# Sparse attention in blocks of 32 queries by 64 keys: tiles, steps and engine order of the attention stage

## The chip, the cores and the metric

The kernel runs on one core of one Trainium2 chip. The metric is the device time of one execution in microseconds. Times of the trace count from its first instruction.

## The reference

The program computes three layers one after another: a masked attention, a mixture of experts with a skip decision, and a feed-forward layer. The change touches the attention alone:

```python
# batch 4, heads 8, sequence S = 576, head_dim 64, stride 32
scores = (q @ k.T) / sqrt(64)
rel = pos[:, None] - pos[None, :]
mask_local   = (rel >= 0) & (rel < 32)                   # heads 0 to 3
mask_strided = (rel >= 0) & (pos_k % 32 == pos_q % 32)   # heads 4 to 7
scores = where(mask, scores, -1e9); scores -= max(scores)
attn = exp(scores); attn /= sum(attn) + 1e-9
out = attn @ v
```

A query of a local head sees the 32 keys up to its own. A query of a strided head sees the keys of its residue class, 18 positions of 576. After the attention, x is its output of shape 2304x512; each token goes to one of eight experts (512 to 1024 to 512) and then through a layer 512 to 2048 to 512.

## The kernel before

q and k come transposed (partition = head half and head dimension), in two orders: by position for the local heads (q_loc, k_loc), and by residue class for the strided ones (q_str, k_str), so that a class is 18 neighbours. A batch is cut into 12 tiles: six local ones of 96 queries by 128 keys and six strided ones of six or five classes (108x108 or 90x90). Two neighbouring tiles form a twin, and a step does one twin for the four heads of its kind. With four batches there are 24 steps (`STEPS`, `TB` = 6).

The work of a step goes through four engines:

1. TensorE, `scores`: four bf16 matmuls with the identity write the masks into PSUM (L806), and eight fp32 matmuls add the scores (L814). The two head halves hh lie on partitions 0 to 63 and 64 to 127, and so on two row tiles of the array.
2. VectorE, `maxima`: one reduction over PSUM for eight maxima (L604) and their scaling (L606).
3. ScalarE, `exps`: eight activations (L489), one for each tile and head, with the maximum as bias, each followed by a read of the accumulator that gives the sum.
4. VectorE, `inverses` (L611, L613); GpSimd multiplies the weights by the inverse sums, once for each tile (L407).
5. TensorE, `turn`: eight transposes (L827); VectorE copies them to SBUF (`copy_turned`, L620); TensorE, `values`: eight fp32 matmuls with v (L841); ScalarE, `place`, copies the result into XT (L497).

An fp32 matmul appears in the trace as two instructions with a weight load each, a transpose as one.

The order on each engine is written by hand: step s does the scores of s and the turning and values of s - 3 (`LAG` = 3). The first five steps and the last are unrolled; the rest is a hardware loop over batches on each engine. TensorE's order in a round is `turn(s-3)`, `scores(s)`, `values(s-3)`; ScalarE's is `exps(s)`, `place(s-3)`; VectorE's is `copy_turned(s-3)`, `maxima(s)`, `inverses(s-1)`. PSUM has two buffers for the scores, two for the turned weights and two for the values. The inputs have one buffer for each kind; SP loads the next batch's local part when the local steps are scored, and so on, by semaphores. The first q_loc and k_loc come in two pieces, so that the first step needs 192 columns of each only.

When all 24 steps are done, the logits (L868) and the rows of x (L862, L513) follow, then routing, the scatter by GpSimd, the experts and the last layer.

Of the kernel before, what the change touches and what calls it, by code (L numbers as in the profile page):

```python
# [7 lines left out]
F32 = mybir.dt.float32  # L8
# [20 lines left out]
LQ = 96  # L29
LT = S // LQ  # L30
CLASSES = [6, 6, 5, 5, 5, 5]
TILES = [(LQ, P, LQ * t, max(0, LQ * t - STRIDE), False, t) for t in range(LT)]
for _t, _c in enumerate(CLASSES):
    _o = PHASE * sum(CLASSES[:_t])
    TILES.append((PHASE * _c, PHASE * _c, _o, _o, True, _t))
TWINS = [(TILES[i], TILES[i + 1]) for i in range(0, len(TILES), 2)]
TB = len(TWINS)
LB = TB // 2
QMAX = PHASE * max(CLASSES)
# [3 lines left out]
LAG = 3  # L43
# [15 lines left out]
C_ID, C_ML0, C_ML, C_MS, C_UP, C_W8, C_TOK, C_ONE, C_END = 0, 128, 256, 384, 492, 620, 628, 646, 774  # L59
# [7 lines left out]
def program(nc, qT, kT, vl, vs, wg, w1, w2, win, wout, cst, out):  # L67
    with ExitStack() as ctx:
# [22 lines left out]
        k_loc, _, o = at("k_loc", [P, 2, S], F32, o)  # L91
        q_str, _, o = at("q_str", [P, 2, S], F32, o)
        k_str, _, o = at("k_str", [P, 2, S], F32, o)
        v_loc, _, o = at("v_loc", [P, LT, 4 * HD], F32, o)
        v_str, _, o = at("v_str", [QMAX, LT, 4 * HD], F32, o)
# [8 lines left out]
        prob, p_at, o = at("prob", [QMAX, 3, 8 * P], F32, o)  # L104
        probT, _, o = at("probT", [P, 2, 4 * QMAX], F32, o)
# [28 lines left out]
        mask_b, _, _ = at("mask_b", [P, C_UP - C_ML0], BF16)  # L134
        wgs, _, _ = at("wgs", [P, DC, LGW], F32)
        sm, _, _ = at("sm", [P, 3, 32], F32)
# [36 lines left out]
        score_b = [ctx.enter_context(nc.psum_tensor(f"pair{i}", [P, 2, 512], F32)) for i in range(2)]  # L173
        bank = [score_b[0][:, 0, :], score_b[0][:, 1, :]]
        bank += [ctx.enter_context(nc.psum_tensor(f"bank{i}", [P, 512], F32)) for i in range(2, 6)]
        bank += [score_b[1][:, 0, :], score_b[1][:, 1, :]]
        warm_b = bank[0]
        probT_b, out_b = bank[2:4], bank[4:6]
# [14 lines left out]
        qk_loc_in, v_loc_in = sem("qk_loc_in"), sem("v_loc_in")  # L193
        qk_str_in, v_str_in = sem("qk_str_in"), sem("v_str_in")
        zeroed, gate_padded, warm_ready, cast = sem("zeroed"), sem("gate_padded"), sem("warm_ready"), sem("cast")
        qk_first_in, masks_in = sem("qk_first_in"), sem("masks_in")
        scored, maxed, biased, probs_done = sem("scored"), sem("maxed"), sem("biased"), sem("probs_done")
        summed, inverted, normed, turned, turn_copied = sem("summed"), sem("inverted"), sem("normed"), sem("turned"), sem("turn_copied")
# [26 lines left out]

        STEPS = B * TB
        FIRST = LAG + 2
        LOOPS = (STEPS - FIRST) // TB

        def steps(eng, step, lag):  # L230
            for s in range(FIRST):
                step(s, s, 0)
            with eng.Fori(0, LOOPS) as b:
                for i in range(TB):
                    step(FIRST + i, TB * b + (FIRST + i), b)
            for s in range(FIRST + LOOPS * TB, STEPS + lag):
                step(s, s, 0)

# [9 lines left out]
        def x_place(i, b):  # L248

            q, _, q0, _, strided, t = TWINS[i][0]  # L250
            src = out_b[i % 2][:, 0:4 * q].rearrange("d (p r) -> d p r", p=2)
            if strided:
                c0, c = sum(CLASSES[:t]), 2 * CLASSES[t]
                dst = XT[:, 2:4, bass.ds(b * S, S)].rearrange("d p (m r) -> d p r m", r=STRIDE)[:, :, c0:c0 + c, :]
                return dst, src.rearrange("d p (r m) -> d p r m", r=c)
            return XT[:, 0:2, bass.ds(b * S + q0, 2 * q)], src

        @block.sync
        def _(sp):
# [3 lines left out]
            def load_local(b, q0=0, q1=S, k0=0, k1=S, arrived=qk_loc_in):  # L263
                sp.dma_start(q_loc[:, :, q0:q1], qT[b, 0, :, :, q0:q1]).then_inc(arrived, 16)
                sp.dma_start(k_loc[:, :, k0:k1], kT[b, 0, :, :, k0:k1]).then_inc(arrived, 16)

            def load_strided(b):
                sp.dma_start(q_str[:, :, :], qT[b, 1]).then_inc(qk_str_in, 16)
                sp.dma_start(k_str[:, :, :], kT[b, 1]).then_inc(qk_str_in, 16)

            def load_v_local(b):
                sp.dma_start(v_loc[:, :, :], vl[b]).then_inc(v_loc_in, 16)

            def load_v_strided(b):
                t0 = 0
                for c, n in ((6, 2), (5, 4)):
                    r0, r = PHASE * sum(CLASSES[:t0]), PHASE * c
                    sp.dma_start(v_str[0:r, t0:t0 + n, :], vs[b, r0:r0 + r * n].rearrange("(t p) d -> p t d", t=n)).then_inc(v_str_in, 16)
                    t0 += n

            load_local(0, q1=2 * LQ, k1=2 * LQ, arrived=qk_first_in)
            load_local(0, q0=2 * LQ, k0=2 * LQ)
            load_v_local(0)
            sp.dma_start(con[:, C_UP:C_END], cst[:, C_UP:C_END]).then_inc(con_in, 16)
            sp.dma_start(pairs[:, :], cst[0:EXTRA, C_END:C_COLS]).then_inc(pairs_in, 16)
            load_strided(0)
            load_v_strided(0)
            sp.wait_ge(zeroed, ZEROED)
# [767 lines left out]
```

## Time and profile before

| | us |
|---|---|
| median of 3 runs | 704.28 (704.14 to 705.2) |
| the profiled execution | 704.93 |
| its span, first to last instruction | 703.2 |
| PE busy | 657.1 (93%) |
| VectorE busy | 330.2 (47%) |
| ScalarE busy | 229.0 (33%) |
| GpSimd busy | 149.3 (21%) |

Busy shares are averages over the whole program. The attention stage is its first 93 us, and there the shares are others. PE stands for TensorE's matmuls, PEld for its weight loads, DVE for VectorE, ACT for ScalarE, POOL for GpSimd, SPq for the DMA queue of SyncE. PE's busy time contains the modelled end of each matmul, so its groups overlap a little. The granted clock is given as a share of 2.4 GHz.

### The profile page before, as it was taken

Reading aid. Unit: us, or ns where it says so; the run is one execution under the profiler, and the core shown is the slowest. Engines: PE = TensorE matmul, PEld = TensorE weight load, DVE = VectorE, ACT = ScalarE, POOL = GpSimd, SP = SyncE. Lnnn points to the kernel's source line nnn. Section 1 sums busy time; section 2 is a strip of 40 time slices with the busy share of each in tenths; the row PEclk is TensorE's granted clock in tenths of the full one; section 3 lists DMA queues with packets and bytes.
Section 4 is the critical chain, followed back from the end, with each engine's and each line's share of the span. In section 5 each row is a group of like instructions: output and inputs, shape, how many; then the busy total and the mean of one; then the engine's idle time right before and its main releaser. Section 6 shows DMA issues by size and latency. Waiting matters only on the chain.

```text
span 703.2 us, 11023 instructions
## 1 busy us (share of the span) xinstructions
PE 657.1 (93%) x4149; PEld 567.4 (81%) x4149; DVE 330.2 (47%) x614; ACT 229.0 (33%) x693; POOL 149.3 (21%) x163
## 2 busy tenths in 40 slices
PE   7999892299999999989999999999999999999995
PEld 4877762299999999968888888888888888888994
DVE  3877733032111112387445644456445564455653
ACT  4999932032111111122223322233222332222331
POOL 1655506302221222785000200002000020000201
PEclk8999977599999999999999999999999999999998
DMA  8565166693777776222000100001000010000100
GB/s 259 180 214 207 40 255 261 225 394 126 265 263 248 262 264 225 88 94 60 1 1 0 61 1 0 1 0 60 0 0 0 0 60 0 0 0 1 61 1 30
DMA packets 37854, 73.95 MB, mean 105 GB/s; under 512 B 2739, under 2 KB 16224, under 8 KB 37808
## 3 DMA queue, kind: packets, MB, share of 16 engines
q1 hardware_dynamic: 34936, 63.92, 26.3%
q0 software_dynamic: 2880, 9.52, 3.5%
q8 instruction: 24, 0.39, 0.2%
q14 instruction: 14, 0.11, 0.1%
HBM read 63.49 MB, written 9.94 MB: 104 GB/s over the span
## 4 chain that ended last, share of the span: by engine, by line
PE 82%; ACT 6%; DMA 4%; POOL 3%; issue 2%; DVE 2%; SPq 0%; DVEq 0%
PE pair L970 28%; PE pair L983 15%; PE bank L983 12%; PE pair L927 10%; PE bank L937 9%; ACT prob L489 5%; DMA WE<-w 2%; POOL x_sorted L418 2%; PE bank L841 1%; PE bank L827 1%; PE bank L911 1%; PE pair L814 1%; PE bank L868 1%; DMA k_loc<-kT 1%; ACT XT L497 1%
## 5 line engine op out<-in xcount | busy, mean ns | idle before, releaser
L970 PE MATMUL pair<-yh,WIH 128*128 128x512 f32 (+1 forms) x320 | 116.5, 371 | 0.2 <-ACT yh L548 0.2
L970 PE MATMUL pair<-yh,WIL 128*128 128x512 f32 (+1 forms) x320 | 116.3, 370 | 0.0
L572 ACT ACTIVATE cl<-cl,half 128x512 f32<-128x512 f32 (+1 forms) x80 | 54.5, 681 | 187.2 <-DVE cl L768 187.2
L477 POOL DMA_INDIRECT out<-XT,tok x18 | 18.8, 1045 | 351.6 <-DVE XT L756 347.7
L776 DVE TENSOR_TENSOR gl<-gr,gh 128x512 fp32r<-128x512 f32 (+1 forms) x80 | 56.3, 703 | 73.1 <-ACT gh L581 71.9
L768 DVE TENSOR_SCALAR cl<-pair 128x512 f32<-128x512 f32 (+1 forms) x80 | 50.9, 637 | 71.0 <-PE pair L970 70.8
L970 PE MATMUL pair<-yl,WIH 128*128 128x512 f32 (+1 forms) x320 | 79.9, 370 | 2.1 <-DVE yl L747 2.1
L927 PE MATMUL pair<-xw,WE 128*128 128x168 f32 x512 | 75.7, 310 | 0.3 <-DMA WE<-w 0.3
L927 PEld LDWEIGHTS pair<-xw,WE 128*128 128x128 f32 x512 | 74.5, 193 | 0.7 <-DMA WE<-w 0.6
L581 ACT CAST gh<-gr 128x512 fp32r<-128x512 f32 (+1 forms) x80 | 46.3, 578 | 85.7 <-PE bank L983 58.3
L937 PE MATMUL bank<-hid,WE 128*128 128x168 f32 x512 | 74.1, 306 | 0.0
L937 PEld LDWEIGHTS bank<-hid,WE 128*128 128x128 f32 x512 | 73.3, 190 | 0.0
L970 PEld LDWEIGHTS pair<-yh,WIH 128*128 128x128 f32 x320 | 60.8, 190 | 11.3 <-ACT yh L548 0.6
L970 PEld LDWEIGHTS pair<-yh,WIL 128*128 128x128 f32 x320 | 60.7, 190 | 10.6
L489 ACT ACTIVATE prob<-pair,sm 96x128 f32<-96x128 f32 (+2 forms) x192 | 65.7, 419 | 10.5 <-DVE sm L606 9.4
L970 PEld LDWEIGHTS pair<-yl,WIH 128*128 128x128 f32 x320 | 57.0, 189 | 13.0 <-DVE yl L747 3.1
L774 DVE TENSOR_TENSOR gr<-gr,cl 128x512 f32<-128x512 f32 (+1 forms) x80 | 52.6, 657 | 22.6 <-ACT cl L572 22.6
L983 PE MATMUL pair<-WOH,gh 128*128 128x512 f32 x160 | 62.5, 391 | 0.0
L983 PE MATMUL pair<-WOL,gh 128*128 128x512 f32 x160 | 62.4, 390 | 0.0
L983 PE MATMUL pair<-WOH,gl 128*128 128x512 f32 x160 | 62.3, 389 | 0.0
L728 DVE TENSOR_TENSOR ytmp<-bank,gb 128x168 f32<-128x168 f32 x32 | 10.6, 333 | 105.6 <-PE bank L937 105.6
L529 ACT ACTIVATE hid<-pair 128x168 f32<-128x168 f32 x64 | 19.9, 310 | 109.7 <-PE pair L927 109.7
(124 smaller groups left out, 933.7 us busy)
## 6 DMA issues: line engine op xcount, KB each, us to landing
WE<-w SPq DMA_DIRECT2D x16, 2048.0 KB, 9.1
xrow<-x_sorted SPq DMA_DIRECT2D x6, 781.5 KB, 10.5
raw_in<-win SPq DMA_DIRECT2D x16, 256.0 KB, 9.2
raw_out<-wout SPq DMA_DIRECT2D x16, 256.0 KB, 2.5
v_loc<-vl SPq DMA_DIRECT2D x4, 768.0 KB, 5.1
q_str<-qT SPq DMA_DIRECT2D x4, 576.0 KB, 5.8
k_str<-kT SPq DMA_DIRECT2D x4, 576.0 KB, 6.8
q_loc<-qT SPq DMA_DIRECT2D x3, 576.0 KB, 4.6
```

Source lines behind the costliest of these rows:

```text
L477: pool.indirect_dma_start(out, bass.IndirectOffsetOnAxis(tok[:, GT * g + t:GT * g + t + 1], 0), rows_of(g, t), None).then_inc(out_done if ...
L489: last = act.activation(prob[0:q, i % 3, e * kk:(e + 1) * kk], score_b[i % 2][0:q, e // 4, e % 4 * kk:(e % 4 + 1) * kk], ACT.Exp, bias=sm[ ...
L529: act.activation(hid[:, par, f, :], hid_b[f % 2][:, 0:WIN], ACT.Relu).then_inc(h_done, 1)
L572: act.activation(cl[:, 0:n], cl[:, 0:n], ACT.Square, bias=half[:, :], scale=0.5).then_inc(squared, 1)
L581: act.copy(gh[:, f % 2, 0:n], gr[:, 0:n]).then_inc(g_high, 1)
L768: dve.tensor_scalar(cl[:, 0:n], h2_b[f % 2][:, 0:n], -1.0, 1.0, ALU.max, ALU.min).then_inc(clamped, 1)
L774: dve.tensor_tensor(gr[:, 0:n], gr[:, 0:n], cl[:, 0:n], ALU.add).then_inc(g_ready, 1)
L776: dve.tensor_tensor(gl[:, f % 2, 0:n], gr[:, 0:n], gh[:, f % 2, 0:n].bitcast(F32), ALU.subtract).then_inc(g_low, 1)
L927: last = pe.matmul(hid_b[f % 2][:, 0:WIN], WE1[:, par, c, P * f:P * (f + 1)], xw[:, buf, c, :], start=(c == 0), stop=(c == DC - 1))
L937: last = pe.matmul(y_b[c][:, 0:WIN], WE2[:, par, f, P * c:P * (c + 1)], hid[:, par, f, :], start=(f == 0), stop=(f == FEC - 1))
L970: last = pe.matmul(h2_b[f % 2][:, 0:tokens], w[:, c, P * f:P * (f + 1)], x[:, c, 0:tokens], start=(k == 0), stop=(k == 3 * DC - 1))
L983: last = pe.matmul(fin_b[t][:, :], x[:, f % 2, P * t:P * (t + 1)], w[:, f, :], start=(f == 0 and k == 0), stop=(f == FFC - 1 and k == 2))
```

## The change

The attention stage is written anew; what follows it stays.

- Tiles. The local heads work in blocks of 32 queries with 64 keys, the strided heads in strips of three classes (54 queries) with 64 keys. Scores stand in groups of 128 rows by 64 keys: four blocks, or two strips, lie below one another. A step does two such groups (j = 0, 1) for four heads, 128 rows by 512 columns. There are five steps for each batch, 20 in all: two of strips, one with the rest (a pair of strips, the first and the last block, the first and the last class), two of blocks.
- TensorE. A step has 4 mask matmuls of 128 columns, and fp32 matmuls of 64 moved columns for the scores: 16 for strips, 24 for the rest, 32 for blocks. The blocks' outputs lie on four column tiles of 32 rows, the strips' on two of 64, and the head halves on two row tiles. The four transposes are 128x128. The values have 16, 24 or 32 matmuls on 64 partitions, with 54, 18 or 32 moved columns and 64 weight columns; the two key halves j alternate. In the rest step, the scores of the two halves are done one after the other.
- Softmax. VectorE takes the maxima and subtracts them from PSUM into prob; ScalarE does one activation of 128x512; VectorE sums, guards and inverts; GpSimd multiplies once.
- The copy of the turned weights moves from VectorE to ScalarE. Scores have three buffers, the turned weights one, prob and the small values five.
- Loads. All inputs come whole, strided first. v_str has 128 rows, v_loc 8 blocks of 128 rows, v_rest three. The batches' loads are unrolled on SP and ordered by scored and pv_done. Constants and padding writes move into the loads of batches 1 and 2.
- VectorE, ScalarE and GpSimd are unrolled; TensorE's loop goes round three times over five steps.

```diff
+TILES_OF = [
+    [(MASK_S[j], [strip(x, j, x) for x in range(2)]) for j in range(2)],
+    [(MASK_S[j], [strip(2 + x, j, x) for x in range(2)]) for j in range(2)],
+    [(MASK_X[j], rest_of_batch(j)) for j in range(2)],
+    [(MASK_L, [block(t + 2 * j, j, n) for n, t in enumerate(FIRST_BLOCKS[0:4])]) for j in range(2)],
+    [(MASK_L, [block(t + 2 * j, j, n) for n, t in enumerate(FIRST_BLOCKS[4:8])]) for j in range(2)],
+]
+SCORES_IN = [0, 1, 2, 0, 1]
...
 # SP
+            load_qk_strided(0)
+            load_qk_local(0)
+            load_v_strided(0)
+            load_v_rest(0)
             load_v_local(0)
+            for b in range(1, B):
+                done = TB * (b - 1)
+                sp.wait_ge(scored, done + REST_STEP + 1)
+                load_qk_strided(b)
+                if b > 1:
+                    sp.wait_ge(pv_done, done)
+                    load_v_local(b - 1)
+                sp.wait_ge(scored, done + TB)
+                load_qk_local(b)
+                sp.wait_ge(pv_done, done + STRIPS_B + 1)
                 load_v_strided(b)
+                sp.wait_ge(pv_done, done + REST_STEP + 1)
+                load_v_rest(b)
...
 # ScalarE
-                for e in range(8):
-                    last = act.activation(prob[0:q, i % 3, e * kk:(e + 1) * kk], score_b[i % 2][0:q, e // 4, e % 4 * kk:(e % 4 + 1) * kk], ACT.Exp,
-                                          bias=sm[0:q, i % 3, 8 + e:9 + e], scale=SCALE, accum_out=sm[0:q, i % 3, 16 + e:17 + e])
+                act.activation(prob[:, n % SLOTS, :], prob[:, n % SLOTS, :], ACT.Exp, scale=SCALE).then_inc(probs_done, 1)
+            def copy_turned(n):
+                act.wait_ge(turned, n + 1)
+                behind(act, pv_done, n)
+                act.copy(probT[:, :], probT_b[:, :]).then_inc(turn_copied, 1)
+            for s in range(STEPS + LAG):
+                if 0 <= s - 1 < STEPS:
+                    exps(s - 1)
+                if 0 <= s - LAG < STEPS:
+                    copy_turned(s - LAG)
+                    place(s - LAG)
 # VectorE
+                dve.tensor_reduce(small[:, 0:8].rearrange("q (h g) -> q h g", h=2), scores, AX_X, ALU.max).then_inc(maxed, 1)
+                dve.tensor_tensor(prob[:, n % SLOTS, :].rearrange("q (h g k) -> q h g k", g=4, h=2), scores,
+                                  small[:, 0:8]...to_broadcast([P, 2, 4, KEYS]), ALU.subtract).then_inc(lowered, 1)
+                dve.tensor_reduce(small[:, 8:16], prob[:, n % SLOTS, :].rearrange("q (g k) -> q g k", g=8), AX_X, ALU.add).then_inc(summed, 1)
+                dve.tensor_scalar(small[:, 16:24], small[:, 8:16], 1e-9, None, ALU.add).then_inc(guarded, 1)
+                dve.reciprocal(small[:, 24:32], small[:, 16:24]).then_inc(inverted, 1)
 # TensorE
+            def scores_of(i, hh):
+                for j, (mask, _) in enumerate(TILES_OF[i]):
+                    pe.matmul(out.rearrange("q (p j k) -> q p j k", p=2, j=2)[:, :, j], ident_b[:, :], mask_b[:, mask, :].unsqueeze(1).to_broadcast([P, 2, KEYS]), ...)
+                    yield
+                for j, (_, parts) in enumerate(TILES_OF[i]):
+                    for p in range(2):
+                        for x in parts:
+                            yield pe.matmul(out[x.row:x.row + x.queries, col:col + KEYS], queries[half_, p, x.first:x.first + x.queries], keys[half_, p, x.keys:x.keys + KEYS], ...)
+            def values(n, i, b):
+                for p in range(2):
                     for hh in range(2):
+                        for pair in zip(*(parts for _, parts in TILES_OF[i])):
+                            for j, x in enumerate(pair):
+                                last = pe.matmul(out_b[KEYS * hh:KEYS * (hh + 1), j, to:to + x.queries], vv[half_, x.index, HD * h:HD * (h + 1)],
+                                                 probT[half_, from_:from_ + x.queries], start=True, stop=True)
+            def round_of(n, i, b, later, scoring):
+                m, k, c = later
+                if not scoring:
+                    turn(n, i)
+                elif k == REST_STEP:
+                    half_scores(m, k, c, 0)
+                    turn(n, i)
+                    half_scores(m, k, c, 1)
+                else:
+                    turn(n, i)
+                    scores(m, k, c)
+                values(n, i, b)
```

## Rows read from the trace of the kernel before

**Rows 1.** Timeline of PE, 0 to 16 us: start, length, operation
```profile
5.94 0.61 PE L806 MATMUL pair<-mask_b,ident_b 96*96 96x256 bf16 x4 [0.32 <-DMA k_loc<-kT]
9.74 1.09 PE L806 MATMUL pair<-mask_b,ident_b 96*96 96x256 bf16 x4 [2.15 <-DMA k_loc<-kT]
15.73 0.47 PE L827 MATMUL bank<-con,prob 96*128 96x96 f32 x3
```
**Rows 2.** Chain of waits at the stage's end: start, us to the next piece
```profile
92.08 0.77 ACT XT L497
```
**Rows 3.** Busy time by stretch, one batch: us, PE, PEld, DVE, ACT, POOL, clock, DMA, GB/s
```profile
15.70:35.00 19.30, 18.83 (x271) 15.85 (x270) 16.29 (x37) 18.94 (x107) 11.94 (x13) 1.00 0.54 176
```
**Rows 4.** Chain of waits, 17 to 106 us
```profile
17.85 0.94 PE pair L814 x16
...
20.72 0.81 PE pair L814 x16
...
26.10 0.44 PE pair L806 x4
26.54 1.05 PE pair L814 x16
27.59 0.89 PE bank L841 x16
...
49.94 1.58 ACT prob L489 x9
...
100.78 0.44 PE pair L877 x4
```
**Rows 5.** Groups by form, 0 to 140 us: busy us, mean ns
```profile
L407 POOL TENSOR_TENSOR prob<-prob,sm 96x512 f32<-96x512 f32 x24 | 24.5, 1039 | 27.8 <-DVE sm L613 27.8
L604 DVE TENSOR_REDUCE sm<-pair 96x8 f32<-96x1024 f32 x12 | 14.7, 1221 | 13.1 <-PE pair L814 13.1
L604 DVE TENSOR_REDUCE sm<-pair 90x8 f32<-90x720 f32 x8 | 7.2, 900 | 0.3
L513 ACT COPY xrow<-pair 128x512 f32<-128x512 f32 x10 | 5.7, 623 | 0.8 <-PE pair L862 0.8
L497 ACT COPY XT<-bank 128x360 f32 x6 | 5.0, 840 | 0.0
```
**Rows 6.** Groups by form, 230 to 700 us, and the chain's copies in a row
```profile
L572 ACT ACTIVATE cl<-cl,half 128x512 f32<-128x512 f32 x64 | 46.3, 724 | 166.2 <-DVE cl L768 166.2
L774 DVE TENSOR_TENSOR gr<-gr,cl 128x512 f32<-128x512 f32 x64 | 45.7, 715 | 17.2 <-ACT cl L572 17.2
105.77 4.02 ACT xrow L513 x8
```
**Rows 7.** Timeline of PE, transposes of 40 columns at half clock
```profile
137.17 0.65 PE L897 MATMUL bank<-con,xfirst 40*128 40x40 f32 x4
```
**Rows 8.** Timeline of PE, four column tiles at full clock, with their mean
```profile
97.84 1.05 PE L868 MATMUL bank<-XT,wgs 128*32 128x512 f32 x8
L868 PE MATMUL bank<-XT,wgs 128*32 128x512 f32 x4 | 0.6, 592 | 0.0
```
**Rows 9.** Timeline of all engines, 92.85 to 93.05 us
```profile
92.96 0.23 PEld L868 LDWEIGHTS bank<-XT,wgs 128*32 128x32 f32 x8 [1.19 <-issue]
92.99 1.08 PE L868 MATMUL bank<-XT,wgs 128*32 128x512 f32 x4 [0.94 <-ACT XT L497]
```
**Rows 10.** Timeline of ACT, 38.3 to 39.5 us
```profile
38.71 0.86 ACT L497 COPY XT<-bank 128x360 f32 x1
39.26 0.45 ACT L489 ACTIVATE prob<-pair,sm 108x108 f32<-108x108 f32 x1
```
**Rows 11.** DMA issues: KB each, us from issue to landing
```profile
k_str<-kT SPq DMA_DIRECT2D x4, 576.0 KB, 6.8
```
**Rows 12.** Timeline of PE in the last rounds, and busy time by stretch
```profile
84.77 1.01 PE L841 MATMUL bank<-probT,v_str 108*64 108x108 f32 x16 [0.89 <-DVE probT L620]
88.00:92.00 4.00, 3.82 (x38) 3.11 (x35) 1.31 (x4) 0.78 (x1) 0.63 (x1) 0.50 0.00 0
```

More of the change, by code:

```diff
@@ L26, with strip, block, rest_of_batch @@
 MASKED = -1.0e9 / SCALE
[L29 to L39, printed above, removed]
+BLOCK, KEYS = 32, 64
+BLOCKS = S // BLOCK
+STRIP = 3 * PHASE
+PAIR = 2 * STRIP
+FIRST_BLOCKS = [t for t in range(BLOCKS) if t % 4 in (1, 2) and t < BLOCKS - 2]
+TILES = [(BLOCK, P, BLOCK * t, BLOCK * (t - 1)) for t in FIRST_BLOCKS] + [(BLOCK, P, S - BLOCK, S - P)]
+LT = len(TILES)
+LOC = len(FIRST_BLOCKS)
+STRIP_PAIRS = (S - 2 * PHASE) // PAIR
+Part = namedtuple("Part", "row kind first queries keys store index out step")
+def strip(w, j, x):
+    out, step, store, index = (STRIP * x, PAIR, "str", w) if w < STRIP_PAIRS - 1 else (0, STRIP, "rest", 0)
+    return Part(KEYS * x, "s", PAIR * w + PHASE + STRIP * j, STRIP, PAIR * w + PHASE + STRIP - KEYS + KEYS * j, store, index, out, step)
+def block(t, j, n):
+    return Part(BLOCK * n, "l", BLOCK * t, BLOCK, BLOCK * (t - 1), "loc", FIRST_BLOCKS.index(t - 2 * j), BLOCK * n, P)
+def rest_of_batch(j):
+    t, c, out = (BLOCKS - 1) * j, (STRIDE - 1) * j, STRIP * 2
+    return [strip(STRIP_PAIRS - 1, j, 0),
+            Part(KEYS, "l", BLOCK * t, BLOCK, max(0, BLOCK * (t - 1)), "rest", 1, out, BLOCK),
+            Part(KEYS + BLOCK, "s", PHASE * c, PHASE, (S - KEYS) * j, "rest", 2, out + 2 * BLOCK, PHASE)]
+MASK_L, MASK_S, MASK_X = 0, (1, 2), (3, 4)
+STRIPS_A, STRIPS_B, REST_STEP, BLOCKS_A, BLOCKS_B = range(5)
+TILES_OF = [
[6 more added lines that the diff above has]
+SCORES_IN = [0, 1, 2, 0, 1]
+TB = len(TILES_OF)
+STEPS = B * TB
 EXP_AT = 4
@@ L845, in step @@
-            def step(k, s, b):
-                for lag, work in ((LAG, turn), (0, scores), (LAG, values)):
-                    m = s - lag
-                    if isinstance(m, int) and not 0 <= m < STEPS:
-                        continue
-                    work(m, (k - lag) % TB, b + (k - lag) // TB)
-            steps(pe, step, LAG)
+            def scores_of(i, hh):
+                out = score_b[SCORES_IN[i]][:, hh, :]
+                half_ = slice(KEYS * hh, KEYS * hh + KEYS)
+                for j, (mask, _) in enumerate(TILES_OF[i]):
+                    pe.matmul(out.rearrange("q (p j k) -> q p j k", p=2, j=2)[:, :, j], ident_b[:, :], mask_b[:, mask, :].unsqueeze(1).to_broadcast([P, 2, KEYS]),
+                              start=(j == 0), stop=False, skip_group_check=True)
+                    yield
+                for j, (_, parts) in enumerate(TILES_OF[i]):
+                    for p in range(2):
+                        for x in parts:
+                            queries, keys = (q_str, k_str) if x.kind == "s" else (q_loc, k_loc)
+                            col = P * p + KEYS * j
+                            yield pe.matmul(out[x.row:x.row + x.queries, col:col + KEYS], queries[half_, p, x.first:x.first + x.queries], keys[half_, p, x.keys:x.keys + KEYS],
+                                            start=False, stop=(j == 1 and p == 1), skip_group_check=True)
@@ L855, in _ @@
+            with pe.Fori(0, LOOPS) as b:
+                for i in range(TB):
+                    k = i + LAG
+                    round_of(TB * b + i, i, b, (TB * b + k, k % TB, b + k // TB), True)
+            for n in range(LOOPS * TB, STEPS):
+                m = n + LAG
+                round_of(n, n % TB, n // TB, (m, m % TB, m // TB), m < STEPS)
             pe.wait_ge(wg_in, 16)
```

308 lines of the change are left out of this document (146 added, 162 removed).

## The prediction

> **What bounds the kernel now.** I read the busy time by stretch first, then the chain of waits inside the stage that changes, then single groups. Only the attention stage changes. Its first turning of weights starts at 15.73 us and its last copy into XT ends at 92.85 us [rows 1, 2]. In between there are 24 rounds on TensorE, six for each batch. The row of the first batch [rows 3] stands for three stretches of 19.2 to 19.4 us: PE is busy 18.8 us and ScalarE 18.9, VectorE only 16.3 and GpSimd 11.9, with the clock at 2.4 GHz throughout. So two engines are full at once. The chain of waits agrees: it runs through PE groups alone in the first batch, and later mostly through the exponentials of L489 [rows 4]. A change that relieves one of the two wins nothing. This one must relieve both, and must not build a new loop between them.
>
> **What goes.** The tiles of 96x128 and about 96x96 scores become tiles of 128 rows by 64 keys, ten instead of twelve for each batch and head. ScalarE's eight exponentials with their eight accumulator reads (0.35 us a pair, 1.58 for nine entries of the chain [rows 4], so about 2.7 us a round) become one activation of 128x512. No row shows that form; a copy of 128x512 takes 0.62 us by itself and 0.50 in a row (4.02 us for eight), and an activation of that size 0.72 [rows 5, 6]. I take 0.50 as its share in a row, bounds 0.48 and 0.75. VectorE's copy of the turned weights moves to ScalarE: 0.60 us until its result is there [rows 5].
>
> **What PE does per round.** Start to start of a group is readable from the chain: scores of 16 instructions take 1.05, 0.94 and 0.81 us for 128, 108 and 90 moved columns, values 0.89 for 108 [rows 4]. Instructions on two tiles of the array run side by side, so 16 are 8 bursts. The slope is (1.05 - 0.81) / 38 / 8 = 0.8 ns per column and burst, about two cycles of 2.4 GHz, and the rest is 0.21 us (scores) or 0.17 us (values) for changing from one kind of tile to another. I apply it to the new counts. Each fp32 matmul is two instructions.
> - Turning: 4 transposes of 128 columns, 0.44 [rows 4] + 0.06 = 0.50 us.
> - Masks: 4 of 128 bf16 columns, 4 x 0.053 (half of the 0.11 of 256 columns [rows 4]) + 0.10 = 0.32 us.
> - Scores: 64 columns. Strips have 32 instructions on four tiles, blocks 64 on eight. If all tiles run side by side, both are 8 bursts: 8 x 64 x 0.83 ns = 0.43 + 0.21 = 0.64 us. The rest step does the two halves one after the other, 24 instructions each on three tiles, with masks: 1.7 us.
> - Values: only the two row halves alternate. Strips 16 bursts x 54 columns = 0.72 + 0.17 = 0.89; blocks 32 bursts x 32 = 0.85 + 0.17 = 1.02, with a few ns per start 1.05; rest 24 bursts, 0.96 us.
> Loading 64 weight columns should fit under 32 moved ones: at the 1.2 GHz level four transposes with 128 weight columns and 40 moved ones take 0.65 us, less a last one of about 0.32 that is 0.11 us each, which is 128 cycles, so it is the longer of the two and not their sum [rows 7]. The sum over a batch is 2 x 2.35 + 3.2 + 2 x 2.5 = 12.9 us on PE. The count of matmul instructions doubles (per batch 264 to 520); that four tiles of 32 columns do run side by side the rows on L868 show: eight instructions of 512 columns end within 1.05 us, less the last one's 0.59 a burst of four costs 0.43 us [rows 8]. That PE is fed fast enough: 8 weight loads and 4 matmuls that began in a window 0.2 us long came after an empty queue, the loads busy 0.23 us in all with 0.15 for one, so 12 instructions start within some 0.08 us, about 7 ns each, 14 ns a pair of load and matmul [rows 9]. With 14 ns a pair the blocks' scores are 64 x 0.014 + 0.21 = 1.1 instead of 0.64.
>
> **The new loop.** ScalarE now does, in this order, exponentials of step n+2, copy of the turned n, placing of n. Placing waits for the values, and the values for the copy. So from one round's values to the next: PE's results land and ScalarE starts, 0.3 us; placing; exponentials 0.50; copy 0.60; PE starts, 0.1; values less their tail. Placing: 512 elements side by side go like the copies above, and 360 scattered ones take 0.84 us [rows 5], in a row with others 0.55 (38.71 to 39.26) [rows 10]. That gives 0.48 for blocks of 512, 0.80 for two copies of 216 scattered, 0.75 for the three of the rest step. Strips: 0.3 + 0.80 + 0.50 + 0.60 + 0.1 + 0.75 = 3.05; blocks 0.3 + 0.48 + 0.50 + 0.60 + 0.1 + 0.97 = 2.95; rest 3.05. Scoring, turning and masks (1.5 us) lie beside placing, exponentials and copy (1.9), so even 1.1 for the blocks' scores costs nearly nothing. Only in the round that scores the rest step does PE come later, by 0.9 us. Batch: 2 x 3.05 + 3.05 + 2 x 2.95 + 0.9 = 15.95 us.
>
> VectorE: the maximum over 512 is 0.68 us (0.90 for 720, 1.22 for 1024 [rows 5]), the subtraction 0.72 [rows 6], the sum 0.68, three small ones and handoffs 0.5: 2.6 a round, under 3.1, so it is nearly as full as before. GpSimd 1.04 once instead of twice. From a scored step to its weights: 1.4 (maximum and subtraction of the next step) + 1.2 + 1.1 + 0.2, inside two rounds with 0.3 us to spare in the round after the rest step. So little slack will be lost now and then; I add 0.65 us a batch, an estimate: 16.6.
>
> **Start, end, transfers.** Before, the first scores start at 5.94 us on 384 KB and the second at 9.74 [rows 1]. Now the first must wait for con and whole q_str and k_str, 1.4 MB, as much as had to land for the second one; so it begins at about 9.5, at the 1.2 GHz level. The third step waits for q_loc and k_loc, 1.15 MB more at some 326 GB/s (176 at a busy share of 0.54 [rows 3]), to about 13.3. The first weights: 9.5 + 1.8 (scores) + 1.5 + 0.7 + 1.9 (second maximum, then sum and inverse) + 1.2 (GpSimd) = 16.8, turned at 17.0 against 15.73: costs 1.3 us. At the end three rounds have no scores and two no exponentials: 1 us less than full rounds. Transfers grow from 3.65 to 4.2 MB a batch; they used 0.54 to 0.55 of the queues for 19.3 us, so need 12.2 us of 16.6 [rows 3]. The tightest one: q_str and k_str are asked for when the rest step is scored, land up to 7.3 us later (6.8 [rows 11] and 0.5 for the issues) and are wanted 7.7 us later, two rounds and a turning: cost nothing to 1 us a batch, taken at nothing.
>
> **The sum.** 17.0 + 4 x 16.6 - 1.0 = 82.4 us for the end of the stage against 92.85: -10.5 us. What follows hangs on it one to one: L868 starts when the last copy is done [rows 2]. The profiled execution took 704.93 us (span 703.2), the median is 704.28; the difference goes to the median: 693.8.
>
> **Rivals.**
> (a) *Small instructions have a floor, and PE is slower than before.* The rows of attention show no closer average than 37 ns a pair (0.60 us of 0.81 for 16 with 90 columns [rows 4]); the 14 ns are from one short spell. A batch on PE is then 2.5 (turning) + 1.7 (masks) + 2.1 (changes) + 480 pairs x f. It decides from f = 27 ns, where it reaches 19.3. With 32 ns it is 21.7 a batch: 17 + 87 - 1 = 103, 10 us slower, 714; with the whole 37 ns it is 24.3 a batch and 724. Against it speak rows 8 and 9. Chance 0.14.
> (b) *A floor per start below that point.* With a floor of 25 ns, a value that I choose just under (a)'s 27, a batch is 18.3 us, the end at 89 to 90, and the time 701 to 702. Chance 0.12.
> The Trainium skill states such a floor (TensorE: Matmul & The Clock Gate, "Wait — 56ns, not 53.3ns?"): start to start never drops below about 25 ns however few columns move. By that rule (b) holds; the trace differs as far as it goes, 7 ns between starts on different tiles, but no row shows it for a long run.
> (c) *The clock falls.* Through the full rounds PE has 2.4 GHz and hardly a gap; in the last three rounds, where it waits about 1 us before each group of values, it fell to 1.2 GHz [rows 12]. The new rounds have gaps of 0.3 to 0.6 us and move fewer columns, something between the two. Were it low in a third of the stage, rounds there take 4.9 instead of 3.3: +10 us, 704; throughout, 724. Chance 0.12.
> (d) *Transfers or slack.* Inputs late by 1 us a batch and VectorE the bound at 3.5 us a round: 17.5 a batch plus waits, 698 to 701. Chance 0.10.
> (e) That the change does not do what it says: five steps with one activation each are in the code; nothing for it.
>
> **How the numbers follow.** The forecast has 0.52, its own range 688 (a batch of 15.2) to 698. (a) is slower, (c) is slower in half of its cases, (b) and (d) faster. About 0.2% (1.4 us) is what a measurement can tell from none. Faster: 0.52 + 0.12 + 0.10 + 0.03 of (c) = 0.77, within 0.2%: 0.04, slower: 0.19. The range reaches from 687 to 710, into (a) and (c).
>
> **What would show it.** Right: five rounds in some 16 to 17 us; L868 at about 82 us; PE groups of blocks' scores near 0.7 us; PE waiting 0.3 to 0.6 us for the copy before each group of values, ScalarE for the values before placing; PE's clock at 2.4 GHz between 16 and 75 us. Wrong: PE without gaps in rounds longer than 3.8 us (a); starts an even 25 ns apart (b); clock slices at 0.5 (c); waits for q_str, k_str or for VectorE's inverse ahead of turning (d).

## The result and the profile after

| | before | after |
|---|---|---|
| median, same comparison | 704.74 us (704.14 to 705.63, 4 runs) | 712.2 us (710.84 to 714.12, 4 runs) |
| ratio | | 1.0107, 95% interval 1.008 to 1.0133 |
| the profiled execution, its span | 704.93, 703.2 | 712.14, 710.2 |
| first turning starts | 15.73 | 17.38 |
| the router's first matmul starts (L868, now L931) | 92.99 | 100.53 |
| from there to the end of the span | 610.2 | 609.7 |

The forecast was 693.8 us, with a range of 687 to 710. The kernel became slower instead, by 1.1%. The last rows of the table place the whole loss in the attention stage: it ends 7.5 us later than before, and 18 us later than the forecast said. A second comparison (e12 below) gave a ratio of 1.0068 [1.0045, 1.0092].

I read the busy time by stretch first, as before. The first group is the kernel after, batch by batch (us; then busy us and count for PE, PEld, DVE, ACT, POOL; granted clock, DMA share, GB/s). It answers to [rows 3].

```profile
17.38:37.20 19.82, 17.65 (x448) 14.21 (x446) 11.63 (x25) 8.26 (x18) 5.22 (x5) 0.76 0.52 177
37.20:57.00 19.80, 18.28 (x520) 15.11 (x520) 11.61 (x25) 8.82 (x19) 5.22 (x5) 0.84 0.68 237
57.00:77.00 20.00, 18.52 (x524) 15.24 (x520) 11.62 (x25) 8.79 (x19) 5.21 (x5) 0.84 0.61 217
77.00:100.50 23.50, 18.90 (x476) 15.96 (x474) 8.32 (x20) 8.42 (x18) 4.40 (x5) 0.65 0.13 47
```

ScalarE fell from 18.9 us to 8.8 a batch and VectorE from 16.3 to 11.6, so the softmax part did what it should. PE alone is full (18.3 of 19.8 us), with fewer columns to move than before, and its clock was at 2.4 GHz throughout before and is now a mixture of the two levels. So the question is what PE does in that time. The chain of waits of the kernel after answers it: the pieces of work that followed one another without slack. These pieces are one round and the two halves of the rest step's scores in the second batch (start, length to the next piece, engine, tile, line):

```profile
49.94 0.59 PE bank L862 x4
50.52 0.22 PE pair L825 x4
50.75 0.60 PE pair L833 x32
51.35 0.51 issue
51.85 1.45 PE out_pair L884 x62
53.31 0.22 PE bank L825 x2
53.53 1.88 PE bank L833 x20
55.41 0.59 PE bank L862 x4
55.99 0.11 PE bank L825 x2
56.10 2.53 PE bank L833 x20
58.64 2.37 PE out_pair L884 x64
61.01 1.04 PE bank L862 x4
62.05 0.43 PE pair L825 x4
62.48 1.13 PE pair L833 x61
```

Turning (L862) takes 0.59 us, masks (L825) 0.22 and the strips' scores (L833) 0.60: the forecast had 0.50, 0.32 and 0.64. The two halves of the rest step's scores take 1.88 and 2.53 us, against 0.64 each in the forecast. At 56.7, inside the second half, the granted clock fell to 1.2 GHz, and behind it every group costs more: values 2.37, turning 1.04, blocks' scores 1.13. The timeline of PE opens up the first half (start, length with the modelled end, tiles, shapes):

```profile
53.46 0.31 PE L833 MATMUL bank<-k_str,q_str 64*54 64x64 f32 x2
53.70 0.24 PE L833 MATMUL bank<-k_loc,q_loc 64*32 64x64 f32 x1
53.71 0.28 PE L833 MATMUL bank<-k_str,q_str 64*18 64x64 f32 x2
53.78 0.22 PE L833 MATMUL bank<-k_loc,q_loc 64*32 64x64 f32 x1
53.93 0.31 PE L833 MATMUL bank<-k_str,q_str 64*54 64x64 f32 x2
```

The shape behind the line is rows times output rows: 64*54 is a strip of 54 queries, on a tile of 64 columns of the array; 64*32 and 64*18 lie on tiles of 32. The first two strip instructions start at 53.46 and 53.56, the first of the narrow ones at 53.70, the last at 53.78, the next strip at 53.93. Each passage from one tile width to the other costs 0.146 us between starts, though the outputs are different rows, and six instructions take 0.47 us. Two passages are 0.29 of it; in the rest, the second instruction of each pair follows the first on the same tile. In the blocks' scores, where all tiles have one width, 64 instructions take 0.79 us: the instructions of a burst, one on each of the eight tiles, start 6 or 7 ns apart. A half of the rest step has four visits to the 64-wide tiles: 4 x 0.47 = 1.88. At the 1.2 GHz level one passage costs 0.24 us.

The Trainium skill has the rule (TensorEngine Tiling (Array Packing), "Key Properties"): changing the tiling mode, and not merely the tile, drains the engine. The trace agrees and gives it a price, 0.146 us each way. The prediction had such a cost only between groups.

By turnings, the four batches last 23.5, 20.1, 20.0 and 19.6 us (the last to the router's first matmul), where the forecast had 16.6, 16.6, 16.6 and 15.6. That is 6.9 + 3.5 + 3.4 + 4.0 = 17.8 us, and 0.4 for the later start: the whole of the miss. The scores of a rest step lie in each of the first three batches, at its end, and before the first turning, but not in the fourth batch.

### The profile page after: what moved, and what is told of

The parts are those of the page before. It is cut to its first block, busy times and chain, and to the rows that moved or that the text cites. A ratio compares the mean times of both kernels' runs of the same rounds, so it can differ in the third digit from the quotient of the medians.

```text
span 710.2 us, 12419 instructions
## 1 busy us (share of the span) xinstructions
PE 659.3 (93%) x5173; PEld 568.1 (80%) x5173; DVE 315.9 (44%) x570; ACT 188.3 (27%) x361; POOL 125.9 (18%) x135
## 4 chain that ended last, share of the span: by engine, by line
PE 89%; POOL 3%; DMA 2%; DVE 2%; issue 2%; ACT 1%; SPq 0%; DVEq 0%
PE pair L1033 27%; PE pair L1046 15%; PE bank L1046 12%; PE pair L990 11%; PE out_pair L1000 5%; PE bank L1000 5%; PE out_pair L884 3%; PE bank L833 3%; POOL x_sorted L443 2%; PE bank L862 2%; PE pair L833 1%; DMA k_loc<-kT 1%; PE out_pair L931 1%; DVE yl L773 1%; PE bank L974 1%
## 5 line engine op out<-in xcount | busy, mean ns | idle before, releaser
L802 DVE TENSOR_TENSOR gl<-gr,gh 128x512 fp32r<-128x512 f32 (+1 forms) x80 | 54.5, 681 | 73.1 <-ACT gh L615 71.1
L797 DVE TENSOR_SCALAR gr<-pair 128x512 f32<-128x512 f32 (+1 forms) x80 | 50.2, 627 | 0.0
L1046 PE MATMUL bank<-WOH,gh 128*128 128x512 f32 x128 | 49.8, 389 | 0.0
L1046 PE MATMUL bank<-WOL,gh 128*128 128x512 f32 x128 | 49.8, 389 | 0.0
L1046 PE MATMUL bank<-WOH,gl 128*128 128x512 f32 x128 | 49.8, 389 | 0.0
```

What stands on the lines that cost most here:

```text
L797: dve.tensor_scalar(gr[:, 0:n], h2_b[f % 2][:, 0:n], 1.0, -1.0, ALU.max, ALU.add).then_inc(over, 1)
L802: dve.tensor_tensor(gl[:, f % 2, 0:n], gr[:, 0:n], gh[:, f % 2, 0:n].bitcast(F32), ALU.subtract).then_inc(g_low, 1)
L1046: last = pe.matmul(fin_b[t][:, :], x[:, f % 2, P * t:P * (t + 1)], w[:, f, :], start=(f == 0 and k == 0), stop=(f == FFC - 1 and k == 2))
```

## The experiments

Each ratio is to the kernel before, on the same chip in the same comparison. "Low" is the time in the stage (first turning to the router's first matmul) that the record of the granted clock shows at 1.2 GHz; "half" is one half of the rest step's scores at 2.4 GHz. These three columns are read from the one profiled execution of each kernel, and "low" changes from execution to execution: the mean granted clock over the whole program was 0.937 to 0.953 in 13 executions of the changed kernel, 0.946 to 0.957 in ten of e2 (the profiled one had 0.957), 0.953 to 0.974 in six of e3, 0.966 to 0.969 in four of e5 and 0.961 to 0.974 in five of e10 (the profiled one had 0.974).

| kernel | median us | ratio, 95% interval | stage | low | half |
|---|---|---|---|---|---|
| changed | 712.2 | 1.0107 [1.008, 1.0133] | 83.2 | 38.8 | 1.88 |
| e12, the same again | 709.75 | 1.0068 [1.0045, 1.0092] | 79.8 | 32.0 | 1.88 |
| e11, half cut | 703.33 | 0.9995 [0.9961, 1.0029] | 73.9 | 19.3 | 1.29 |
| e1, sorted | 703.67 | 0.9999 [0.9977, 1.0022] | 77.2 | 29.4 | 1.14 |
| e2, narrow | 698.25 | 0.9924 [0.9896, 0.9951] | 70.7 | 16.1 | 0.57 |
| e3, filler | 708.67 | 1.0053 [1.0009, 1.0096] | 80.8 | 10.3 | 1.88 |
| e4, values | 708.17 | 1.0053 [1.0017, 1.0088] | 76.3 | 28.6 | 1.88 |
| e5, narrow and filler | 693.57 | 0.983 [0.9776, 0.9885] | 68.8 | 6.5 | 0.57 |
| e8, narrow and values | 696.74 | 0.9876 [0.9822, 0.9931] | 70.4 | 26.1 | 0.57 |
| e6, narrow and swap | 699.25 | 0.9927 [0.9902, 0.9953] | 73.1 | 21.9 | 0.57 |
| e9, narrow, unrolled | 705.84 | 1.0014 [0.9975, 1.0053] | 77.0 | 29.2 | 0.57 |
| e10, narrow, filler, values | 689.73 | 0.9817 [0.9768, 0.9866] | 66.2 | 0.0 | 0.57 |

**e1: the strips first, then the narrow parts.** One change of width inside a half instead of seven.

```diff
-                for j, (_, parts) in enumerate(TILES_OF[i]):
+                rest = len(TILES_OF[i][0][1]) == 3
+                for turn_ in range(2 if rest else 1):
+                    for j, (_, parts) in enumerate(TILES_OF[i]):
...
-                        for x in parts:
+                            for x in ((parts[1:] if turn_ else parts[:1]) if rest else parts):
```

> The changed kernel with one edit: in each half of the rest step's scores, the four strips (54 rows, 64-wide tile) come first and then the eight blocks and single classes (32-wide tiles), instead of strip, block, single four times. The same matmuls. Theory A (each change between a 64-wide and a 32-wide tile empties the array: 0.146 us at 2.4 GHz, eight in each half): one change less than twice is left, a half falls from 1.88 to about 1.1 us, a batch loses 1.5 to 2 us at full clock and more where the clock was low: 712 falls to 702 to 706. Rival B (PE's clock falls because few columns move, whatever the order): the half falls, but the clock stays low a third of the stage, 707 to 710. Rival C (the loop over ScalarE or VectorE's order sets the rounds): less than 2 us.

The half fell from 1.88 to 1.14 us, as expected, and the kernel is level with before. The instructions are the same, so the order alone was worth 0.7% (against e12) to 1.1% (against the first comparison). The half is still twice that of e2 below, and one passage of 0.15 us is not the reason. All eight strip instructions of a half lie on one tile, and there they start 56 ns apart:

```profile
52.21 0.65 PE L835 MATMUL bank<-k_str,q_str 64*54 64x64 f32 x8
52.79 0.24 PE L835 MATMUL bank<-k_loc,q_loc 64*32 64x64 f32 x1
```

The stage of 77.2 us holds something else as well. PE stopped for 2.3 us inside the values of a block step, with no engine named that it waited for (`29.11 ... [2.30 <-issue]`), and the clock was at 1.2 GHz from 28.7 to 42.4. The first batch took 24.2 us by that; the second and third took 17.1 and 16.1.

**e2: the rest step's strips cut to 32 and 22 queries.** All tiles have one width; the count of matmuls rises.

```diff
+            def cut(parts):
+                if len(parts) != 3:
+                    return parts
+                wide = parts[0]
+                return [wide._replace(queries=BLOCK),
+                        wide._replace(row=wide.row + BLOCK, first=wide.first + BLOCK, queries=wide.queries - BLOCK)] + parts[1:]
...
-                        for x in parts:
+                        for x in cut(parts):
```

> The changed kernel with one edit: in the rest step's scores each strip of 54 queries is cut into 32 and 22, so that all outputs lie on 32-wide tiles and no change of tile is left inside a half; 8 matmul instructions more in each half. Theory A: a half takes 8 bursts, 0.45 to 0.6 us instead of 1.88, a batch loses 2.6 us or more, and the clock, low after each rest step, falls less often: 694 to 702. Rival B (clock falls because few columns move): rounds no shorter elsewhere, clock low even more, 704 to 710. Rival C (ScalarE's loop or VectorE's order): under 3 us gained.

PE's chain in the kernel with cut strips:

```profile
61.47 0.57 PE bank L840 x30
62.74 0.57 PE bank L840 x30
68.89 2.62 issue
```

A half is now 0.57 us although it has a third more instructions; the forecast had 0.64. The kernel is faster than before. Its batches take 18.3, 16.5, 15.2 and 20.7 us, where the forecast had 16.6, 16.6, 16.6 and 15.6. So the passages explain the first three batches for the most part, and nothing of the fourth. The last row above stands at the end of the third batch: a stop of PE inside a group of 64, described under e9. The clock was low from 72.6 us to the end of the stage.

**e11: the cut for j = 0 only.** A dose between the two: two visits to the wide tiles in a half.

```diff
-                        for x in parts:
+                        for x in (parts if j else cut(parts)):
```

> A dose: the rest step's strips cut to 32 and 22 queries for j = 0 only, so that about four changes of tile size stand inside a half instead of eight or none. Theory (each change costs 0.15 us by itself): a half takes about 0.57 + 4 x 0.15 = 1.2 us at the full clock, 1.4 to 1.7 at the lower; the time lies between the uncut and the cut kernel, about 703 to 706 us. Rival (the half is slow because three tiles with rows of 54 queries are slow, not because of changes): a half near the mean of 1.88 and 0.57 too, but with even starts and not with gaps of 0.15 at the changes. Rival (the loss comes from the first change alone or from the clock): a half of 1.7 us or more, 709 to 712.

Timeline of PE of this kernel, the second half of a rest step's half (start, length, shapes):

```profile
64.37 0.22 PE L840 MATMUL bank<-k_loc,q_loc 64*32 64x64 f32 x1
64.52 0.32 PE L840 MATMUL bank<-k_str,q_str 64*54 64x64 f32 x2
64.76 0.24 PE L840 MATMUL bank<-k_loc,q_loc 64*32 64x64 f32 x1
64.77 0.28 PE L840 MATMUL bank<-k_str,q_str 64*18 64x64 f32 x2
64.84 0.22 PE L840 MATMUL bank<-k_loc,q_loc 64*32 64x64 f32 x1
64.99 0.32 PE L840 MATMUL bank<-k_str,q_str 64*54 64x64 f32 x2
```

Within one half, narrow instructions follow each other at once and every wide one is set apart by 0.15 us on both sides. No visit gives 0.57, two give 1.29, four give 1.88: 0.36 and 0.33 us a visit. The median went along: 698, 703, 710 to 712. That excludes "three tiles are slow", since the pauses stand only where the width changes.

**e3: extra matmuls on the changed kernel.** They compute nothing that is used and keep PE busy before each turning.

```diff
+                for _ in range(4 if (i + LAG) % TB == REST_STEP else 2):
+                    pe.matmul(probT_b[:, :], ident_b[:, :], mask_b[:, 0:4, :].unsqueeze(1).to_broadcast([P, 2, 4, KEYS]), start=True, stop=True, skip_group_check=True)
```

> The changed kernel with matmuls added that nobody reads: 2 of 512 bf16 columns before each turning, 4 in the round that scores the rest step (0.21 us each at 2.4 GHz). The rest step keeps its tile changes. Theory B (the low clock is what costs): PE's clock stays at 2.4 GHz through the stage, the added 0.4 to 0.9 us a round lie mostly in its waits, 704 to 708. Theory A: the tile changes stay, the clock is repaired but the rounds get longer by what is added, 709 to 716.

The time at 1.2 GHz in the stage fell from 38.8 to 10.3 us. Still the kernel stays slower than before: some 45 extra matmuls of 0.22 us or more are in PE's order (2003 instructions in the stage, against 1959), and one rest round waited 1.5 us for k_loc. The median lies between what the two theories expected, and its interval overlaps that of the changed kernel. What the clock gives back and what the extra matmuls cost are not separated by this run; it shows that with the passages left in, the two together buy little.

**e5: e2 and e3 together.**

> The rest step's strips cut into 32 and 22 as in the second experiment (698.25 us, stage of 70.7 us, PE's clock low for 16 us of it), plus 2 matmuls of 512 bf16 columns that nobody reads before each turning and 4 in the round that scores the rest step. Theory A (the tile changes were the cost, and the low clock followed from them): the clock was already high in the loop, so the added columns can win only at the stage's end, where it still fell, and cost up to 0.4 us in the rounds that PE sets: 696 to 701. Rival B (the low clock is a cost of its own all through): 690 to 695.

Here the same extra matmuls gain: 0.983 against e2's 0.9924, the range of rival B. The gain lies where the clock had been low in e2: the batches last 19.4, 16.3, 16.3 and 16.9 us, so the fourth is 3.8 us shorter than in e2 and the others are no shorter on the whole. Part of that is a stop at the loop's end of 1.1 us instead of 2.6. The median, 693.57, is close to the forecast by chance: it is another kernel.

**e4: the head halves of the values inside the loop over parts.** Four tiles alternate instead of two.

```diff
-                    for hh in range(2):
-                        for pair in zip(*(parts for _, parts in TILES_OF[i])):
+                    for pair in zip(*(parts for _, parts in TILES_OF[i])):
+                        for hh in range(2):
```

> The changed kernel with one edit: the values' loop has the head halves inside the loop over parts, so that four tiles of 64x64 alternate instead of two. Instructions on one tile follow one another no closer than 58 ns in the trace of the changed kernel, with 54 as with 32 moved columns. If the 58 ns belong to the tile, the blocks' values fall from 1.4 to about 1.1 us and the strips' from 0.66 to 0.6, on the loop over ScalarE: 1 to 4 us less, 708 to 711. If they belong to the engine, no change.

Values of a block step at 2.4 GHz, first of the changed kernel, then of e4, in the timeline of PE:

```profile
51.85 1.45 PE L884 MATMUL out_pair<-probT,v_loc 64*64 64x32 f32 x64 [0.51 <-issue]
```
```profile
50.60 1.14 PE L884 MATMUL out_pair<-probT,v_loc 64*64 64x32 f32 x64 [0.51 <-issue]
```

The group shrank by 0.3 us, yet the ratio, 1.0053, overlaps that of the changed kernel (1.0107 and 1.0068): a gain is likely but not resolved. **e8** is the same on top of e2:

> Cut strips as above, and the values' loop with the head halves inside, so that four tiles alternate. With the long scores gone the values lie on the loop over ScalarE (placing, exponentials, copy, values): blocks' values 1.45 to about 1.1 us, strips' and the rest's less by 0.1 to 0.3, so 0.3 us a round: 6 us less, 692 to 695. If VectorE's order sets the rounds: under 2 us, 696 to 699.

Its interval overlaps e2's as well, and the median of 696.74 lies in the range expected for the case that the values do not set the rounds. The 26.1 us at 1.2 GHz, against 16.1 in e2, are no sign of anything: the profiled execution had the lowest mean clock of e8's four (0.946), that of e2 the highest of its ten.

**e6: VectorE takes the inverses of the step before ahead of the maxima,** on top of e2.

```diff
-                if s < STEPS:
-                    maxima(s)
                 if s >= 1:
                     inverses(s - 1)
+                if s < STEPS:
+                    maxima(s)
```

> Cut strips as above, and VectorE takes the sums and inverses of step s-1 before the maxima of step s instead of after. In the second experiment's trace the turning of the rest step waited for maxima, subtraction, sum, inverse and GpSimd in a row (51.3 to 54.9 us, a round of 5.5 us against 2.4 to 2.9 of the others), because the sum of the rest step stands behind the maxima of the next. If that order is the cost, the long round falls to 3 us and the time by 2 to 8 us, to 690 to 696. If ScalarE's loop or PE sets the rounds, nothing changes (697 to 699); if the maxima now come late behind the exponentials, it is slower, 700 to 706.

The idea came from the kernel after, where the turning at 67.26 waits for this chain behind the rest step:

```profile
63.63 0.70 DVE sm L636
64.36 0.69 DVE prob L639
65.05 0.60 DVE sm L645
65.68 0.18 DVE sm L647
65.88 0.21 DVE sm L649
66.16 1.05 POOL prob L434
67.26 0.66 PE bank L862 x4
```

With the swap the round that scores the rest step took 4.3 us twice. In e2 it took 5.5 and 4.2, but the 5.5 held a wait of 1.3 us for k_loc, so nothing was gained. Of the other rounds of a batch, two rose from 2.8 and 2.9 us to 3.4 and 3.2, since the exponentials now wait for a later subtraction. The full batches take 16.1 us, against 15.2 in e2's third, which had no wait for inputs. The ratio does not differ from e2's.

**e9: TensorE's loop written out,** on top of e2, to remove the stop of 2.62 us where the loop ends.

```diff
-            with pe.Fori(0, LOOPS) as b:
-                for i in range(TB):
...
-            for n in range(LOOPS * TB, STEPS):
+            for n in range(STEPS):
```

> Cut strips as above, and PE's loop over batches written out, so that all its waits have constant values and its code is about twice as long. In the second experiment PE stood still for 2.6 us inside a group of scores at 68.9 us, just where its loop ends, and a 16 KB block of instructions was fetched at 69.2. If the fetch after the loop is the cost, that gap goes; but twice the code must then be fetched while the loads run: 696 to 697 if the fetches keep ahead, 700 to 710 if PE then starves in every round.

PE in the timeline of the unrolled kernel, and the row of the instruction queue on the page of e2 and of the unrolled kernel (transfers, MB, share):

```profile
36.01 0.82 PE L840 MATMUL pair<-k_loc,q_loc 64*32 64x64 f32 x61
40.47 0.42 PE L840 MATMUL pair<-k_loc,q_loc 64*32 64x64 f32 x3 [3.64 <-issue]
56.14 0.57 PE L840 MATMUL pair<-k_loc,q_loc 64*32 64x64 f32 x35
60.66 0.67 PE L840 MATMUL pair<-k_loc,q_loc 64*32 64x64 f32 x29 [3.96 <-issue]
```
```profile
q8 instruction: 28, 0.46, 0.3%
```
```profile
q8 instruction: 36, 0.59, 0.3%
```

The stop at the loop's end is gone, and two of 3.6 and 4.0 us have come. In each of these stops the trace names no engine that PE waited for, and an instruction transfer of q8 ran (at 38.2 and 58.1 us here, at 69.2 in e2). PE went on 1.3 to 1.7 us after the transfer had ended. So I take it that PE waited for its code; the trace does not name that wait. The clock fell to 1.2 GHz inside both stops here (at 39.0 and 59.5 us). The Trainium skill describes such fetches in blocks of 16 KiB (Runtime: NRT & Kernel Launch, "Instruction fetch mechanics"); 0.46 MB in 28 transfers agrees. In e2, no q8 transfer began between 32.5 us and 69.2, and PE made no such stop from 32 to 68 us, which fits a loop whose second and third pass need no new code. Written out, the kernel loses 0.9% against e2.

**e10: cut, extra matmuls and four alternating tiles together.**

> The changed kernel with three edits at once: the rest step's strips cut to 32 and 22 queries (no change of tile size inside a half), the head halves of the values inside the loop over parts (four tiles alternate instead of two), and two matmuls of 512 columns with no use before each turning, four in the round that scores the rest step. Theory (the changes inside the rest step, then the fallen clock, then the values' floor): the edits act on different terms. Cutting with the extra matmuls gave 0.983 of before, the values alone another 0.995 beside the changed kernel: so 0.975 to 0.983, 688 to 693 us, granted clock low in less than 8 us of the stage. Rival (ScalarE's loop or VectorE's chain is now the bound, PE has room): no gain over 693, batches stay at 16.2 us.

Busy time by stretch of this kernel, batch by batch:

```profile
30.50:46.50 16.00, 14.54 (x545) 11.78 (x545) 11.74 (x25) 8.93 (x19) 5.34 (x6) 1.00 0.86 282
46.50:62.50 16.00, 15.46 (x553) 12.48 (x551) 11.74 (x25) 8.81 (x19) 5.07 (x6) 1.00 0.84 283
```

It is the fastest kernel of the study in the median, 1.8% below before and inside the range expected, and in the profiled execution the clock never fell in the stage. Batches last 18.8, 16.2, 15.4 and 15.7 us, and the stage ends at 80.9, where the forecast had 82.4. What follows the stage takes 606.9 us there, 2 to 4 us less than in the other kernels; 2 us of it are the logits, which took 4.4 us at 2.4 GHz and 6.5 in e2. The value order's own share over e5 is within the intervals. In the second row PE is busy 15.5 of 16 us, a good part of it with the extra matmuls.

**e12: the changed kernel again,** to compare on this chip.

> The changed kernel itself, unaltered, beside the others on the same chip. If nothing but the chip differs: 1.008 to 1.013 of before, stage of 80 to 84 us, a half of the rest step's scores 1.9 us at the full clock and 2.4 to 2.9 at the lower, granted clock low in 30 to 40 us of the stage.

It confirms the loss, at the lower end of what was expected; the stage was 79.8 us here, with 32 us at 1.2 GHz.

## Why the prediction was wrong

**The step that failed** is "The rest step does the two halves one after the other, 24 instructions each on three tiles, with masks: 1.7 us". It gave a half 0.43 + 0.21 = 0.64 us, as if changing the kind of tile happened only between groups. The row for that change was at hand (0.17 and 0.21 us of each group in [rows 4]); what I did not do was to walk through the inner loop, `for x in parts`, and see that in this one step it alternates strip, block, strip end. A half measured 1.88 us, and 2.4 to 2.97 at the lower clock. Twice 1.24 us at 2.4 GHz is 2.5 of the 3.4 us that the second and the third batch lack. e1, e11 and e2 show it from three sides. With the passages gone (e2), the stage ends at 85.5 us, against 100.5 and 98.1 of the changed kernel: 12.6 to 15 of the 18 us.

**The second part is rival (c), in part as a consequence.** The clock fell to 1.2 GHz in or right behind each rest step (at 32.8, 56.7 and 77.2 us, and from 8.9 to 22.6 around the first one), and once more at 90.9 in the last rounds, where PE waits 1.4 and 0.8 us for copies, as before in [rows 12]. In e12, the same kernel, it fell at 52.1, 76.0 and 89.6, and not at the rest step ahead of 35; so a half of this kind does not bring the fall every time. I had expected gaps of 0.3 to 0.6 us to matter; what stands before the falls at the rest steps is a half in which PE starts six instructions per 0.47 us. By the records PE is busy there, and it does little. In e2, with the passages gone, there is no fall at a rest step, and the time at 1.2 GHz in the profiled execution was 16.1 us instead of 38.8 and 32.0, without any further edit. The mean clocks of all executions, given above the table of the experiments, move the same way, but their ranges overlap. With extra matmuls it was 6.5 and 0.0 (e5 and e10), worth another 0.9% (e5 against e2). Before, the stage had 5.6 us of it.

**The third part is the end of the stage,** which the sum had as 1 us less than full rounds, although [rows 12] showed the lower clock there. The fourth batch took 19.6 us, and 20.7 in e2 (a stop of 2.6 us included), against 15.6. Where the clock stayed at 2.4 GHz (e10) it took 15.7.

**Smaller terms.**
- Values: forecast 1.05 for blocks, 0.89 for strips; measured 1.45 and 0.66. A burst over four tiles came every 58 ns in e10 (64 instructions in 0.93 us), whether 32 or 54 columns move. So the slope of 0.8 ns per column read from [rows 4] does not continue to 32 columns, and the argument that loading 64 weight columns hides under 32 moved ones did not hold as a price; what sets the 58 ns no run shows. With two alternating tiles the 64 instructions take 1.39 us to the next group's start, with four 1.07. Cost to blocks 0.4 us a round, hidden partly in ScalarE's loop.
- Code: not in the prediction at all. With PE's instructions doubled, the kernel after has stops of 0.9 us (at 29.4) and 0.6 us (at 87.1) without a named cause, e1 one of 2.3 us (at 26.8) and e2 one of 2.6 us (at 68.9). The kernel before has none of that kind in the stage: the waits that its trace lists for PE all name the engine that ended them.
- Transfers, rival (d): in the kernel after PE never waited for them once the turnings had begun. In others it did once: 1.5 us for k_loc in e3, 1.3 in e2, 0.56 in e10. Tight, as forecast, and at the local inputs and not at q_str.

**What came out by luck.** The first turning was forecast at 17.0 and measured at 17.38, but on another path. The first scores began at 7.98 us and not at 9.5, and the first weights were ready at 14.2 and not at 16.8. PE then spent the time until 17.38 in the first rest step's scores, whose halves took 3 us each at 1.2 GHz:

```profile
11.78 0.46 PE L833 MATMUL bank<-k_str,q_str 64*54 64x64 f32 x2
17.04 0.40 PE L833 MATMUL bank<-k_str,q_str 64*18 64x64 f32 x2
17.38 1.11 PE L862 MATMUL bank<-con,prob 128*128 128x128 f32 x4
```

In e2 the first turning starts at 14.8, and it waits for the weights. Two errors of about 2.5 us cancelled.

**What was right.** The copies and VectorE's operations: 0.58, and 0.68, 0.69, 0.68 us alone. The activation takes 0.63 us, over the 0.50 taken and inside its bounds. The second and third batch once the passages were gone: 15.2 to 16.5 us in e2, e5 and e10, against 15.95 + 0.65. Rivals (a) and (b), a floor per small instruction, which held 0.26 of the chance, are refuted for the scores: 64 instructions over eight tiles started within 0.79 us, an average of 12 ns, down to 6. The values, on two tiles, came 20 ns apart on average. The floor of 25 ns that the prediction cited (the Trainium skill, TensorE: Matmul & The Clock Gate) does not hold between different tiles here. The rest of the program took as long as before, 609.7 against 610.2 us.

What stays open: how much of the first batch's excess (23.5 us, against 20 of the others) is the lower clock and how much code. In e10, with the clock at 2.4 GHz throughout, the first batch was still 2.7 to 3.4 us longer than the next two, and PE stood still there several times for 0.4 to 0.8 us with no engine named, so much of that part looks like code. That each stop waits for code is inferred from the transfers beside it.

## What to carry to other kernels

Price an inner loop on TensorE by walking through its instructions in order and counting how often the width of the column tile changes, not by group: each passage cost 0.146 us here, as much as twelve instructions of the blocks' scores. Count also how many instructions in a row fall on one tile. A busy record is no proof of work: six instructions in 0.47 us read as a full PE, and the clock fell there. When a change doubles the number of small instructions, look for stops without a waited-for engine beside transfers of the instruction queue; here the body kept in the loop was the faster one. Ask of a term that came out right whether its path did too: the first turning was on time for a wrong reason.

## What the hardware did that I had not expected

- A change between column tiles of 64 and of 32: 0.146 us between starts at 2.4 GHz, 0.24 at 1.2, each way, also between tiles that do not overlap.
- With tiles of one width, fp32 instructions on different tiles start 6 to 7 ns apart in runs of eight, and 64 of them in 0.79 us. On one tile they started 56 ns apart (e1). A burst on four tiles with 64 weight columns came every 58 ns, for 32 as for 54 moved columns (e10).
- PE stood still 2.6 us at a loop's end, and up to 4.0 us in the same code written out, each time beside a transfer of 16 KB of instructions and with no engine named. In e9 the clock fell inside both stops.
- Two matmuls of 512 columns with no use before each turning, four in the round that scores the rest step, made the cut kernel faster: 0.983 [0.9776, 0.9885] against 0.9924 [0.9896, 0.9951].
